# Attention scores from two row groups of the array instead of zero-padded key copies

## The chip, the cores and the metric

The kernel runs on one core of a Trainium2 chip. A core has TensorE (PE, matrix products), VectorE (DVE), ScalarE (ACT), GpSimd (POOL) and SyncE (SP, which here issues nearly all transfers). They run side by side and meet through semaphores. The metric is the device time of one execution in microseconds, the median of several.

## The reference

Three stages, all in fp32. `cur` is linear attention with a decaying state, for 2 batches, 8 heads, 768 positions and head size 48; its result goes as 1536 tokens of 384 features through a gated layer with 8 experts (hidden size 1024, top one, capacity 384) and then through a dense layer of hidden size 2048 with a squared relu.

```python
for t in range(S):
    kt, vt, rt = (k[:, :, t], v[:, :, t], r[:, :, t])
    cur = np.einsum('bhd,bhe->bhde', u[None] * kt, vt)
    y[:, :, t] = np.einsum('bhd,bhde->bhe', rt, state + cur)
    state = w[None, :, :, None] * state + np.einsum('bhd,bhe->bhde', kt, vt)
...
h = np.maximum(np.einsum('ecd,edf->ecf', disp, w1), 0.0)
y = np.einsum('ecf,efd->ecd', h, w2)
...
out = (np.maximum(x @ w_in, 0.0) ** 2) @ w_out
```

## The kernel before

**The attention loop.** The sequence is cut in chunks of C = 128 positions. A loop of three iterations with four steps each (`SLOTS = 4`) goes over 12 chunks, n = 0 to 11, that alternate between the two batches. The 8 heads stand as G = 4 pairs: of a pair g, head o=0 lies in partitions 0 to 47 and head o=1 in partitions 64 to 111 (`D = 48`, `ODD = 64`, `ROWS = 112`); the partitions between hold zeros. Each step works in a slot of its own for its inputs; `am`, `ps_a0`, `ps_a1`, `ps_y` and `ps_kv` exist once, `Kb` and `vb` twice.

One step n does this, engine by engine:

- SP stores the result of chunk n-4, waits for that store to land (`x_stored`), and then issues the loads of chunk n: `feat` (queries and keys by feature), `vT`, `rk` and `vx` (L280 to L283). The first four chunks and two weight pieces are issued ahead of the loop, and SP's queue is in order.
- POOL multiplies the keys in `feat` by their decay in place (L360, `k_decayed`), then the queries into `Rd` (L361, `r_decayed`), then makes `khat` (L367) and `ru` (L369).
- ACT copies the keys of the two heads of each pair to `Kb` (`kb_ready`), where the other head's rows stay zero; then the gate's logits to `vx`, the values to `vb`, and the decayed state to `Sd`.
- PE computes the values' gate products (L427, 3 matmuls), the scores (L433, 8 matmuls of 112 rows, 128x128 each, pair by pair), the state update `ps_kv` (L441, 4 matmuls) and the output `ps_y` (L449 and L451, 12 matmuls: state part, then one masked score block per head, accumulated).
- DVE masks each bank of scores into `am` (L795, with the triangle `before`), makes `ru`, `csum` and `cv` (L799 to L802), adds `ps_y` and `cv` into `x_sb` (L805) and `heads_l` (L806), updates the state (L811) and sums the router's logits (L814).

A bank of scores holds four blocks of 128 columns. Before, bank 0 holds both heads of pairs 0 and 1, bank 1 both heads of pairs 2 and 3. PE signals `scored` after each bank, DVE signals `masked` after each, and the y phase waits for the first before pairs 0 and 1 and for the second before pairs 2 and 3. All matmuls are in fp32; each appears in the trace as two instructions. Engines run their instructions in program order, and the next step's gate products and scores are behind this step's y phase on PE.

**After the loop** DVE, PE and POOL compute the routing (L830 on), POOL gathers the tokens of each expert from `attention_out`, and the expert stage and the dense stage follow, on weights streamed by SP.

Ahead of the loop DVE and POOL each clear one `Kb`, and ACT's loop waits for both (`kb_cleared`).

Of the kernel before, what the change touches and what calls it, by code (L numbers as in the profile page):

```python
# [20 lines left out]
P = 128  # L21
F32 = mybir.dt.float32
# [8 lines left out]
B, H, S, D = 2, 8, 768, 48  # L31
# [3 lines left out]
C = 128  # L35
NC_ = S // C
NT = B * NC_
G = H // 2
ODD = 64
ROWS = ODD + D  # L40
# [18 lines left out]
def build(nc, feat_d, vT_d, rk_d, vx_d, w_d, u_d, wg_d, wts_d, xd, out):  # L59
    with ExitStack() as ctx:  # L60
        def sem(name):
            return ctx.enter_context(nc.semaphore(name))

        def sb(name, shape, dt=F32, scope=ctx):
            return scope.enter_context(nc.sbuf_tensor(name, shape, dt))
# [30 lines left out]
        start = sb("start", [P, E])  # L96
# [13 lines left out]
        with ExitStack() as a:  # L110
            feat = [sb(f"feat{u}", [P, 2, G * C], F32, a) for u in range(SLOTS)]
            rk = [sb(f"rk{u}", [P, 2, DM], F32, a) for u in range(SLOTS)]
            vx = [sb(f"vx{u}", [P, H, DX], F32, a) for u in range(SLOTS)]
            vT = [sb(f"vT{u}", [P, KT, C], F32, a) for u in range(SLOTS)]
            Rd = [sb(f"Rd{u}", [P, G * C], F32, a) for u in range(SLOTS)]
            Kb = [sb(f"Kb{u}", [P, G, 2, C], F32, a) for u in range(2)]
            vb = [sb(f"vb{u}", [P, G, 2, 2 * DX], F32, a) for u in range(2)]
            khat = [sb(f"khat{u}", [P, G, P], F32, a) for u in range(SLOTS)]
            ru = [sb(f"ru{u}", [P, DM], F32, a) for u in range(SLOTS)]
            x_sb = [sb(f"x_sb{u}", [P, DM], F32, a) for u in range(SLOTS)]  # L120
            am = sb("am", [P, 2, G * C], F32, a)
            csum = sb("csum", [P, H], F32, a)
            cv = sb("cv", [P, H, DX], F32, a)
            heads_l = sb("heads_l", [P, H, E], F32, a)
            St = [sb(f"St{b}", [P, G, 2 * DX], F32, a) for b in range(B)]
            Sd = sb("Sd", [P, G, 2 * DX], F32, a)
            T = sb("T", [P, G, 256], F32, a)
            Tk = sb("Tk", [P, G, C], F32, a)
            Tr = sb("Tr", [P, G, C], F32, a)
            iw = sb("iw", [P, G], F32, a)  # L130
            wcol = sb("wcol", [P, G], F32, a)
            tokw = sb("tokw", [P, G, P], F32, a)
            ub = sb("ub", [P, DM], F32, a)
# [15 lines left out]
        ps_a = [ps_a0, ps_a1]  # L149
# [25 lines left out]

        k_decayed = sem("k_decayed")
        r_decayed = sem("r_decayed")
        kb_cleared = sem("kb_cleared")
        kb_ready = sem("kb_ready")
        sd_ready = sem("sd_ready")  # L180
        khat_ready = sem("khat_ready")
        ru_ready = sem("ru_ready")
# [3 lines left out]
        scored = sem("scored")  # L186
        masked = sem("masked")
# [68 lines left out]
        def chunk_view(ap):  # L256
            return ap.rearrange("p (g s) -> p g s", g=G)
# [68 lines left out]
        def _(pool):  # L326
# [10 lines left out]
            def iota(dst, pattern, base, mult):  # L337
# [13 lines left out]
            steps.after(nc.gpsimd.memset(earlier[:, :, :], 1.0))  # L351
            nc.gpsimd.affine_select(out=earlier[:, :, :], in_=earlier[:, :, :], compare_op=ALU.is_gt, fill=0.0, base=0,
                                    pattern=[[1, E], [-1, E]], channel_multiplier=0).then_inc(consts, 1)
            nc.gpsimd.memset(Kb[1][:, :, :, :], 0.0).then_inc(kb_cleared, 1)
            pool.wait_ge(table_ready, 1)
            with pool.Fori(0, NC_ // 2) as i:
                for u in range(SLOTS):
# [52 lines left out]
        def _(pe):  # L410
# [3 lines left out]
            for g in range(G):  # L414
                mm = pe.transpose(ps_kv[:, g * P:g * P + ROWS], Tr[0:ROWS, g, :], ident[0:ROWS, 0:ROWS])
# [4 lines left out]
            with pe.Fori(0, NC_ // 2) as i:  # L420
                for u in range(SLOTS):
                    n, b = 4 * i + u, u % 2

                    pe.wait_ge(in_vT[u], 16 * (i + 1))
                    pe.wait_ge(vx_ready, n + 1)
                    for k in range(KT):
                        mm = pe.matmul(ps_x[:, 0:H * E], vT[u][:, k, :], wg[:, k, :], start=(k == 0), stop=(k == KT - 1))  # L427
                    mm.then_inc(vwg_psum, 1)
                    pe.wait_ge(kb_ready, 2 * n + 2)
                    pe.wait_ge(r_decayed, n + 1)  # L430
                    for g in range(G):
                        for o in range(2):
                            mm = pe.matmul(ps_a[g // 2][:, (2 * (g % 2) + o) * C:(2 * (g % 2) + o + 1) * C],  # L433
                                           Kb[u % 2][0:ROWS, g, o, :], Rd[u][0:ROWS, g * C:(g + 1) * C], start=True, stop=True)
                        if g % 2:
                            mm.then_inc(scored, 1)
                    pe.wait_ge(khat_ready, n + 1)
                    pe.wait_ge(vx_ready, n + 2)
                    pe.wait_ge(state_ready, 2 * n + 2)
                    for g in range(G):  # L440
                        mm = pe.matmul(ps_kv[0:ROWS, g * 2 * DX:(g + 1) * 2 * DX], khat[u][:, g, 0:ROWS],  # L441
                                       vx[u][:, 2 * g:2 * g + 2, :].rearrange("p o d -> p (o d)"), start=True, stop=True)
                    mm.then_inc(kv_done, 1)
                    pe.wait_ge(vb_ready, 2 * n + 2)
                    for g in range(G):
                        if g % 2 == 0:
                            pe.wait_ge(masked, 2 * n + g // 2 + 1)
                        pair = ps_y[:, g * 2 * DX:(g + 1) * 2 * DX]
                        pe.matmul(pair, Rd[u][0:ROWS, g * C:(g + 1) * C], St[b][0:ROWS, g, :], start=True, stop=False)  # L449
                        for o in range(2):  # L450
                            mm = pe.matmul(pair, am[:, g // 2, (2 * (g % 2) + o) * C:(2 * (g % 2) + o + 1) * C],  # L451
                                           vb[u % 2][:, g, o, :], start=False, stop=(o == 1))
                    mm.then_inc(y_done, 1)

# [4 lines left out]
            for j in range(1, NT + 1):  # L459
                mm = pe.matmul(ps_pos[:, 0:nt], ones_b[:, :], oh[:, NT - j:2 * NT + 1 - j, :].rearrange("p t e -> p (t e)"),  # L460
                               start=False, stop=(j == NT))
            mm.then_inc(pos_psum, 1)

            for t in range(NT):
                pe.wait_ge(onehot, t + 1)
                mm = pe.matmul(ps_tab[:, 0:2 * E * CT], onehb[:, t, :], tokb[:, t, :, :].rearrange("p a s -> p (a s)"),
                               start=(t == 0), stop=(t == NT - 1))
# [55 lines left out]
            for q in range(CT):  # L523
                pe.wait_ge(first_gathered[q], 16)
                for k in range(KT):
                    mm = pe.transpose(ps_e[k][:, q * P:(q + 1) * P], xg[0][:, q, k * P:(k + 1) * P], ident[:, :])
# [94 lines left out]
        def _(act):  # L621
            def copy(dst, src):
                return nc.scalar.activation(dst, src, ACT.Copy)  # L623
# [1 line left out]
            act.wait_ge(tokw_psum, 1)  # L625
            copy(tokw[:, :, 0:ROWS], chunk_view(ps_kv[:, :])[:, :, 0:ROWS]).then_inc(tokw_ready, 1)

            act.wait_ge(kb_cleared, 2)
            with act.Fori(0, NC_ // 2) as i:
                for u in range(SLOTS):  # L630
                    n, b = 4 * i + u, u % 2

                    act.wait_ge(k_decayed, n + 1)
                    for o in range(2):
                        rows = slice(ODD * o, ODD * o + D)
                        copy(Kb[u % 2][rows, :, o, :], chunk_view(feat[u][rows, 1, :])).then_inc(kb_ready, 1)
                    act.wait_ge(in_tok[u], 32 * (i + 1))
                    act.wait_ge(vwg_psum, n + 1)
                    copy(vx[u][:, :, D:DX], ps_x[:, 0:H * E].rearrange("p (h e) -> p h e", h=H)).then_inc(vx_ready, 1)
                    act.wait_ge(vx_ready, n + 2)  # L640
                    act.wait_ge(vb_cleared, 2)
                    values = vx[u][:, :, :].rearrange("p (g o) d -> p g o d", o=2)
                    for o in range(2):
                        copy(vb[u % 2][:, :, o, o * DX:(o + 1) * DX], values[:, :, o, :]).then_inc(vb_ready, 1)

                    act.wait_ge(state_ready, 2 * n + 2)
                    for g in range(G):
                        nc.scalar.activation(Sd[0:ROWS, g, :], St[b][0:ROWS, g, :], ACT.Copy,
                                             scale=T[0:ROWS, g, 192:193]).then_inc(sd_ready, 1)
# [94 lines left out]
        def _(dve):  # L744
            v = nc.vector
# [4 lines left out]

            v.memset(T[w, :, 64:65], 1.0)
            v.memset(oh[:, :, :], 0.0).then_inc(vx_ready, 1)
            v.memset(Kb[0][:, :, :, :], 0.0).then_inc(kb_cleared, 1)
            dve.wait_ge(in_w, 16)
            v.tensor_copy(T[w, :, 65], wcol[w, :]).then_inc(dve_step, 1)
            v.reciprocal(T[w, :, 63], wcol[w, :]).then_inc(dve_step, 1)
# [3 lines left out]
            while m <= 128:  # L760
                top = min(64 + 2 * m, 255)
                n = top - 64 - m
# [26 lines left out]
            with dve.Fori(0, NC_ // 2) as i:  # L789
                steps.enter(i, 5 * SLOTS)  # L790
                for u in range(SLOTS):
                    n, b = 4 * i + u, u % 2
# [16 lines left out]
                    for o in range(2):  # L809
                        rows, cols = slice(ODD * o, ODD * o + D), slice(DX * o, DX * o + DX)  # L810
# [228 lines left out]
```

## Time and profile before

| | us |
|---|---|
| median of 3 runs | 480.9 |
| lowest and highest run | 480.21, 481.16 |
| profiled execution, from its first to its last instruction (span) | 477.0 |
| PE busy in the span | 433.4 |
| DVE busy | 294.8 |
| ACT busy | 218.9 |
| POOL busy | 119.7 |

The profiled execution's own time is given as its span alone; the median of the runs is 3.9 us above it. The profile lists instructions with their start and duration, and for an idle engine what it waited for. Each group of matmuls on PE is pipelined, so the rows of consecutive groups overlap by the time that one instruction takes to pass; what counts is the distance of the starts. The granted clock is a share of 2.4 GHz.

### The profile page before, as it was taken

What the parts mean: (1) busy time and instruction counts of PE and PEld (TensorE: products, weight loads), DVE (VectorE), ACT (ScalarE), POOL (GpSimd) and SP (SyncE); (2) the same over time, 40 slices, a digit from 0 to 9 for tenths busy, and PEclk for the clock granted to TensorE, in tenths of its full rate; (3) what the DMA queues carried; (4) which work ended last, traced back from release to release, by engine and by line L of the source; (5) the groups of instructions that cost most, each with busy time, mean ns of one, the idle gap of its engine ahead of it and who ended that gap; (6) DMA issues with size and microseconds to landing.
All of it is one profiled execution on the core that took longest, in us unless ns stands there. A gap on an engine that the chain in (4) does not pass through costs nothing.

```text
span 477.0 us, 8640 instructions
## 1 busy us (share of the span) xinstructions
PE 433.4 (91%) x2933; PEld 408.4 (86%) x2934; DVE 294.8 (62%) x490; ACT 218.9 (46%) x382; POOL 119.7 (25%) x114
## 2 busy tenths in 40 slices
PE   2998989525999999999999999999999999999993
PEld 2998988514999999999899889898998989899892
DVE  8888877689467666676666574554635455553431
ACT  2554544321456647556555463444544345544320
POOL 6955765556940220220000000000300000300003
PEclk9999999955899999999999999999999999999998
DMA  7966576770375475465354423232522313400001
GB/s 212 299 219 207 172 239 209 287 264 26 117 234 191 156 226 196 159 223 198 135 198 154 181 88 111 71 129 67 160 104 81 117 66 132 133 0 1 0 0 67
DMA packets 20989, 69.51 MB, mean 146 GB/s; under 512 B 3352, under 2 KB 9769, under 8 KB 20960
## 3 DMA queue, kind: packets, MB, share of 16 engines
q1 hardware_dynamic: 18656, 64.40, 41.5%
q0 software_dynamic: 2304, 4.73, 2.7%
q8 instruction: 18, 0.29, 0.2%
q14 instruction: 11, 0.09, 0.1%
HBM read 64.39 MB, written 7.08 MB: 150 GB/s over the span
## 4 chain that ended last, share of the span: by engine, by line
PE 76%; DMA 9%; DVE 6%; issue 3%; SPq 3%; POOL 1%; ACT 0%; ACTq 0%; DVEq 0%; POOLq 0%
PE bank L482 36%; PE bank L501 21%; PE bank L491 14%; DMA attention_out<-x_sb 8%; PE bank L473 1%; DVE osb L894 1%; PE bank L433 1%; DMA vx<-in_vx 1%; PE bank L451 1%; DVE r_q L848 1%; SPq L280 1%; SPq L281 1%; SPq L282 1%; SPq L283 1%; DVE r_q L847 0%
## 5 line engine op out<-in xcount | busy, mean ns | idle before, releaser
L900 DVE TENSOR_TENSOR wlo<-raw,whi 128x1536 fp32r<-128x1536 f32 x53 | 93.2, 1758 | 99.9 <-ACT whi L623 99.6
L623 ACT ACTIVATE whi<-raw 128x1536 fp32r<-128x1536 f32 x56 | 83.1, 1488 | 85.3 <-PE bank L501 46.7
L403 POOL DMA_INDIRECT out<-osb,oidx x12 | 12.9, 1076 | 246.2 <-ACT osb L735 243.8
L501 PE MATMUL bank<-whi,hhi 128*128 128x384 f32 x192 | 64.7, 337 | 0.2 <-DVE hlo L919 0.2
L501 PE MATMUL bank<-whi,hlo 128*128 128x384 f32 x192 | 64.7, 337 | 0.0
L501 PE MATMUL bank<-wlo,hhi 128*128 128x384 f32 x192 | 64.6, 336 | 0.0
L482 PE MATMUL bank<-yhi,wlo 128*128 (+1 forms) x144 | 56.9, 395 | 0.0
L482 PE MATMUL bank<-yhi,whi 128*128 (+1 forms) x144 | 56.8, 394 | 0.0
L482 PE MATMUL bank<-ylo,whi 128*128 (+1 forms) x144 | 56.8, 394 | 0.0
L482 PE MATMUL bank<-xshi,whi 128*128 128x256 f32 x192 | 55.3, 288 | 1.1 <-DVE xslo L904 0.9
L491 PE MATMUL bank<-hhi,whi 128*128 128x256 f32 x192 | 55.5, 289 | 0.2 <-DVE ylo L949 0.2
L482 PE MATMUL bank<-xslo,whi 128*128 128x256 f32 x192 | 54.5, 284 | 0.9 <-issue 0.9
L482 PE MATMUL bank<-xshi,wlo 128*128 128x256 f32 x192 | 54.3, 283 | 0.0
L491 PE MATMUL bank<-hlo,whi 128*128 128x256 f32 x192 | 53.6, 279 | 0.0
L491 PE MATMUL bank<-hhi,wlo 128*128 128x256 f32 x192 | 53.6, 279 | 0.0
L676 ACT ACTIVATE rl<-bank 128x512 f32<-128x512 f32 x48 | 28.6, 601 | 53.8 <-PE bank L482 53.8
L915 DVE TENSOR_TENSOR sq<-rl 128x512 f32<-128x512 f32 x48 | 32.9, 688 | 29.9 <-ACT rl L676 29.9
L389 POOL DMA_INDIRECT xg<-attention_out,gidx x24 | 24.8, 1034 | 74.0 <-PE bank L473 60.6
L482 PEld LDWEIGHTS bank<-xshi,whi 128*128 128x128 f32 x192 | 36.8, 192 | 2.6 <-DVE xslo L904 2.1
L482 PEld LDWEIGHTS bank<-xslo,whi 128*128 128x128 f32 x192 | 36.9, 192 | 1.1 <-issue 1.1
L501 PEld LDWEIGHTS bank<-whi,hhi 128*128 128x128 f32 x192 | 36.1, 188 | 1.6 <-issue 0.6
L501 PEld LDWEIGHTS bank<-wlo,hhi 128*128 128x128 f32 x192 | 36.1, 188 | 1.0
(153 smaller groups left out, 861.2 us busy)
## 6 DMA issues: line engine op xcount, KB each, us to landing
raw<-in_wts SPq DMA_DIRECT2D x56, 768.0 KB, 4.3
feat<-in_feat SPq DMA_DIRECT2D x12, 448.0 KB, 3.9
rk<-in_rk SPq DMA_DIRECT2D x12, 384.0 KB, 4.5
vx<-in_vx SPq DMA_DIRECT2D x12, 224.0 KB, 5.2
vT<-in_vT SPq DMA_DIRECT2D x12, 192.0 KB, 3.8
attention_out<-x_sb SPq DMA_DIRECT2D x12, 192.0 KB, 4.6
out<-xg SPq DMA_DIRECT2D x12, 192.0 KB, 2.3
xg<-attention_out,gidx POOLq DMA_INDIRECT x24, 3.6
```

The lines of the kernel that those rows point to most:

```text
L280: sp.dma_start(feat[u][0:ROWS, :, :], feat_d[b, bass.ds(c, 1)].rearrange("a p k n -> (a p) k n")).then_inc(in_feat[u], 16)
L281: sp.dma_start(vT[u][:, :, :], vT_d[b, bass.ds(c, 1)].rearrange("a p k s -> (a p) k s")).then_inc(in_vT[u], 16)
L282: sp.dma_start(rk[u][:, :, :], rk_d[b, bass.ds(c, 1)].rearrange("a s k n -> (a s) k n")).then_inc(in_tok[u], 16)
L389: nc.gpsimd.indirect_dma_start(out=xg[e % 2][:, q, :], out_offset=None, in_=xd[:, :], in_offset=bass.IndirectOffsetOnAxis(ap=gidx[:, e * C ...
L403: nc.gpsimd.indirect_dma_start(out=out[:, :], out_offset=bass.IndirectOffsetOnAxis(ap=oidx[:, t:t + 1], axis=0), in_=osb[:, t, :], in_offs ...
L482: mm = pe.matmul(banks[ft][:, 0:width], w[:, r, cols], x(k), start=(k == 0 and step == 0), stop=(k == KT - 1 and step == 2))
L491: mm = pe.matmul(ps_e[dt][:, 0:width], w[:, r, cols], x[:, par, ft, 0:width], start=(q == 0 and ft == 0 and step == 0), stop=(q == EQ - 1 ...
L501: mm = pe.matmul(ps_o[tt][:, 0:DM], x[:, par, ft, tt * P:(tt + 1) * P], w[:, r, cols], start=(v == 0 and ft == 0 and step == 0), stop=(v = ...
L623: return nc.scalar.activation(dst, src, ACT.Copy)
L676: nc.scalar.activation(rl[:, ft, :], banks[ft][:, :], ACT.Relu).then_inc(h_relu, 1)
L900: v.tensor_tensor(wlo[:, r, :], raw[:, r, :], whi[:, r, :].bitcast(F32), ALU.subtract).then_inc(w_lo, 1)
L915: v.tensor_tensor(sq[:, ft, :], rl[:, ft, :], rl[:, ft, :], ALU.mult).then_inc(h_sq, 1)
```

## The change

The scores of the head o of a pair are computed from its own 48 rows alone: the stationary operand is the keys in `feat` and the moving one `Rd`, both cut to rows 0 to 47 or 64 to 111. Bank o now holds the heads o of all four pairs, and the mask and the y phase read the blocks by that order. `Kb`, ACT's two copies a step and the two clears go. PE waits for POOL's `k_decayed` itself, both `scored` signals come at the last pair, and the y phase waits for both masks before its first matmul.

```diff
-            Kb = [sb(f"Kb{u}", [P, G, 2, C], F32, a) for u in range(2)]
...
-            nc.gpsimd.memset(Kb[1][:, :, :, :], 0.0).then_inc(kb_cleared, 1)
...
-                    pe.wait_ge(kb_ready, 2 * n + 2)
+                    pe.wait_ge(k_decayed, n + 1)
                     pe.wait_ge(r_decayed, n + 1)
                     for g in range(G):
                         for o in range(2):
-                            mm = pe.matmul(ps_a[g // 2][:, (2 * (g % 2) + o) * C:(2 * (g % 2) + o + 1) * C],
-                                           Kb[u % 2][0:ROWS, g, o, :], Rd[u][0:ROWS, g * C:(g + 1) * C], start=True, stop=True)
-                        if g % 2:
-                            mm.then_inc(scored, 1)
+                            rows = slice(ODD * o, ODD * o + D)
+                            mm = pe.matmul(ps_a[o][:, g * C:(g + 1) * C], feat[u][rows, 1, g * C:(g + 1) * C],
+                                           Rd[u][rows, g * C:(g + 1) * C], start=True, stop=True)
+                            if g == G - 1:
+                                mm.then_inc(scored, 1)
...
                     pe.wait_ge(vb_ready, 2 * n + 2)
+                    pe.wait_ge(masked, 2 * n + 2)
                     for g in range(G):
-                        if g % 2 == 0:
-                            pe.wait_ge(masked, 2 * n + g // 2 + 1)
                         pair = ps_y[:, g * 2 * DX:(g + 1) * 2 * DX]
                         pe.matmul(pair, Rd[u][0:ROWS, g * C:(g + 1) * C], St[b][0:ROWS, g, :], start=True, stop=False)
                         for o in range(2):
-                            mm = pe.matmul(pair, am[:, g // 2, (2 * (g % 2) + o) * C:(2 * (g % 2) + o + 1) * C],
+                            mm = pe.matmul(pair, am[:, o, g * C:(g + 1) * C],
                                            vb[u % 2][:, g, o, :], start=False, stop=(o == 1))
...
-            act.wait_ge(kb_cleared, 2)
...
-                    act.wait_ge(k_decayed, n + 1)
-                    for o in range(2):
-                        rows = slice(ODD * o, ODD * o + D)
-                        copy(Kb[u % 2][rows, :, o, :], chunk_view(feat[u][rows, 1, :])).then_inc(kb_ready, 1)
...
-            v.memset(Kb[0][:, :, :, :], 0.0).then_inc(kb_cleared, 1)
```

## Rows read from the trace of the kernel before

**Rows 1.** The page: chain of work that ended last, by engine and by line

```profile
PE 76%; DMA 9%; DVE 6%; issue 3%; SPq 3%; POOL 1%; ACT 0%; ACTq 0%; DVEq 0%; POOLq 0%
PE bank L482 36%; PE bank L501 21%; PE bank L491 14%; DMA attention_out<-x_sb 8%; PE bank L473 1%; DVE osb L894 1%; PE bank L433 1%; DMA vx<-in_vx 1%; PE bank L451 1%; DVE r_q L848 1%; SPq L280 1%; SPq L281 1%; SPq L282 1%; SPq L283 1%; DVE
```

**Rows 2.** SP's queue in order of time: start us, us, operation

```profile
19.19 0.36 SPq L288 DMA_DIRECT2D attention_out<-x_sb  x1
28.28 0.35 SPq L280 DMA_DIRECT2D feat<-in_feat  x1
...
30.46 0.35 SPq L288 DMA_DIRECT2D attention_out<-x_sb  x1
...
79.11 0.34 SPq L280 DMA_DIRECT2D feat<-in_feat  x1
```

**Rows 3.** SP's waits up to 100 us: total us, times, longest

```profile
SPq L280 <- DMA attention_out<-x_sb: 39.4, 8, 8.5
```

**Rows 4.** DVE in order of time: start, steps 1 and 2, 6, 11

```profile
2.48 0.17 DVE L755 COPY T<-wcol 112x4 f32<-112x4 f32 x1 [0.32 <-DMA wcol<-in_w]
...
24.36 0.56 DVE L805 TENSOR_TENSOR x_sb<-bank,cv 128x384 f32<-128x384 f32 x1
...
26.42 1.29 DVE L795 TENSOR_TENSOR am<-bank,before 128x512 f32<-128x512 f32 x2
...
30.30 0.56 DVE L805 TENSOR_TENSOR x_sb<-bank,cv 128x384 f32<-128x384 f32 x1 [0.79 <-PE bank L451]
...
56.44 0.56 DVE L805 TENSOR_TENSOR x_sb<-bank,cv 128x384 f32<-128x384 f32 x1
...
86.76 0.69 DVE L795 TENSOR_TENSOR am<-bank,before 128x512 f32<-128x512 f32 x1 [0.72 <-PE bank L433]
...
91.19 0.56 DVE L805 TENSOR_TENSOR x_sb<-bank,cv 128x384 f32<-128x384 f32 x1 [1.04 <-PE bank L451]
```

**Rows 5.** POOL in order of time, steps 0 and 11

```profile
5.71 1.50 POOL L360 TENSOR_TENSOR feat<-feat,Tk 112x512 f32<-112x512 f32 x1 [1.00 <-DMA feat<-in_feat]
...
82.93 1.27 POOL L360 TENSOR_TENSOR feat<-feat,Tk 112x512 f32<-112x512 f32 x1 [2.44 <-DMA feat<-in_feat]
84.16 1.26 POOL L361 TENSOR_TENSOR Rd<-feat,T 112x512 f32<-112x512 f32 x1
```

**Rows 6.** ACT in order of time, step 11

```profile
84.23 1.28 ACT L623 ACTIVATE Kb<-feat 48x512 f32<-48x512 f32 x2 [3.71 <-POOL feat L360]
```

**Rows 7.** PE in order of time, step 11

```profile
85.56 2.05 PE L433 MATMUL bank<-Rd,Kb 112*128 112x128 f32 x16 [0.94 <-ACT Kb L623]
87.45 0.95 PE L441 MATMUL bank<-vx,khat 128*112 128x112 f32 x8
88.24 0.39 PE L449 MATMUL bank<-St,Rd 112*128 112x112 f32 x2
```

**Rows 8.** PE in order of time, step 2, which waits for no load

```profile
24.09 0.79 PE L427 MATMUL bank<-wg,vT 128*128 128x64 f32 x6
24.72 2.00 PE L433 MATMUL bank<-Rd,Kb 112*128 112x128 f32 x16
26.56 0.95 PE L441 MATMUL bank<-vx,khat 128*112 128x112 f32 x8
```

**Rows 9.** PE in order of time, the first step

```profile
11.02 3.73 PE L433 MATMUL bank<-Rd,Kb 112*128 112x128 f32 x16
14.54 1.10 PE L441 MATMUL bank<-vx,khat 128*112 128x112 f32 x8
15.47 0.39 PE L449 MATMUL bank<-St,Rd 112*128 112x112 f32 x2
```

**Rows 10.** Windows (us): engines' busy time, granted clock, DMA share, GB/s

```profile
26.00:28.00 2.00, 2.00 (x21) 2.00 (x20) 1.85 (x4) 1.95 (x6) 1.28 (x2) 1.00 0.37 146
28.00:29.00 1.00, 1.00 (x11) 1.00 (x10) 0.84 (x3) 0.42 (x1) 0.00 (x0) 1.00 0.00 0
```

**Rows 11.** A window at the start of the expert stage

```profile
120.00:124.00 4.00, 3.86 (x20) 3.86 (x21) 0.93 (x5) 0.39 (x2) 3.69 (x3) 0.58 0.60 239
```

More of the change, by code:

```diff
@@ L177, in build @@
         r_decayed = sem("r_decayed")
-        kb_cleared = sem("kb_cleared")
-        kb_ready = sem("kb_ready")
         sd_ready = sem("sd_ready")
```

## The prediction

> **What bounds the kernel now.** I read the page first, its chain of work, to see where the changed loop stands in the whole [rows 1]. TensorE holds 76% of the chain, but nearly all of that is the expert and MLP stage, where the change touches nothing. The attention loop ends at about 91 us of 477.0, and its own entry in the chain is a transfer: the stores of attention_out take 8% of the span. The second view is SyncE's queue in order of time, and who it waits for [rows 2, 3]. From the first finished chunk on, SP does the same round eight times: issue the store of chunk n, wait for its landing, issue the four loads of chunk n+4, go on to store n+1. It waited 39.4 us for landings in 8 waits, 4.9 each. The rounds run from 19.19 to 79.11, 7.5 us apart on average ((79.11 - 19.19)/8). The results are ahead of SP: that of chunk 1 was there at 24.9 (its x_sb began at 24.36 [rows 4]) and SP came to it at 30.46; that of chunk 6 was there at 57.0, and at the mean round SP comes to it some ten microseconds later. So in the middle of the loop the compute engines follow the loads, and a faster or slower step there buys or costs nothing so long as the results stay ahead of SP.
>
> That leaves two places where a step still counts. One is the last chunk, n=11. Its features were issued at 79.11, and POOL decayed keys and queries from 82.93 to 85.42 [rows 5]. ACT copied the keys to Kb until 85.51 [rows 6], the first score matmul began at 85.56, kv at 87.45, the first y matmul at 88.24 [rows 7], and DVE took the result at 91.19 [rows 4]. What follows (routing, gather, experts) hangs on that moment. The other is the period of a step that does not wait for a load, since a backlog could reach the last chunk. The steady step shows it: x_sb began at 24.36 and 30.30, a period of 5.94 us [rows 4]. TensorE is full in it (gate 0.63, scores 1.84, kv 0.78, y the remaining 2.69; starts from [rows 8]), and DVE's own circle is as long: x_sb to the first mask 2.06 us, then about 0.69 for half of the masking, then y.
>
> **The change part by part.** *Kb's copies go.* ACT's two copies, 1.28 us a step, ended 0.09 us after POOL had Rd ready (85.51 against 85.42 [rows 5, 6]). The step can begin only that much sooner, 0.08 us (85.56 becomes about 85.48), because POOL's second multiplication is late next. ACT's freed time buys nothing more: it holds 0% of the chain [rows 1].
>
> *The two clears of Kb go* (128x1024 on DVE and on POOL ahead of the loop). Behind its clear DVE still sat 0.32 us idle for the transfer of `wcol` [rows 4], and POOL 1.00 us for the first features [rows 5], so I cost both at nothing; without that cover each is worth what a clear takes, 0.9 us. SP's queue and all transfers stay as they are.
>
> *The scores.* The number of matmuls stays: 8 a step, in the trace 16 instructions. Before, they are 0.118 us apart (87.45 - 85.56 over 16) and one lasts d = 2.05 - 15 x 0.118 = 0.28 us [rows 7]. What half the rows cost, no row shows: every matmul of the trace uses 112 or 128 rows. The two ends: (a) the two heads' instructions do not overlap, pitch 0.118 as before; (b) two heads run at once, a pair of matmuls per 0.236 us where it was 0.47. The nearest rows speak for both. Gate matmuls stream 64 columns, half of the scores' 128, and still come every 0.105 us [rows 8] (0.63/6); so something other than the streaming, presumably the weight load ahead of each, keeps 0.10 us per instruction, and if loads of the two row groups stand in one line, (a) holds. Against that, the two groups share neither rows nor a bank. I take (b), narrowly, and keep (a) for the range.
>
> The Trainium skill, TensorEngine Tiling (Array Packing), Key Properties, says that different tiles can load and multiply in parallel, which would be (b); no row here shows it. TensorE: Matmul & The Clock Gate, LDWEIGHTS, of the same Trainium skill, says that a load costs by its columns and not by its rows; the 0.105 us at 64 streamed columns agrees with a floor of that sort, and by that rule alone the sum would be that of (a).
>
> *The masks.* Before, the first bank held four head blocks and was complete after half of the scores, so DVE masked it while TensorE wrote the second. Now the heads alternate and the bank of the first heads is complete only at the 14th of 16 instructions; and y waits for both masks where it waited for one. Before, the first mask began 0.09 us after the eighth instruction's end (85.56 + 7 x 0.118 + 0.28 = 86.67, mask at 86.76 [rows 4]). Two masks back to back take 1.29 us [rows 4] (26.42). From the end of a copy to the waiting matmul it is 0.05 us (85.51 to 85.56). Behind the waiting y stand y's 24 instructions and the next chunk's gate and scores; DVE's x_sb waits for them.
>
> The last step then:
> - (b): 85.48 + 3 x 0.236 + 0.118 + 0.28 + 0.09 = 86.68; masks to 87.97; y at 88.02, against 88.24. Gain 0.2 us. kv no longer stands between, it runs beside the masks: POOL's khat is there at about 86.6, kv's 0.79 end at 87.4.
> - (a): 85.48 + 13 x 0.118 + 0.28 + 0.09 = 87.38; masks to 88.67; y at 88.72. Loss 0.5 us.
>
> The break-even pitch lies between, nearer to (b): 0.7 us of scores saved are met by 0.5 us of masking that was hidden.
>
> *The first step* works on a slower TensorE: 16 instructions in 3.52 us, 0.22 apart, d = 3.73 - 15 x 0.22 = 0.43 [rows 9]. Under (b) the first x_sb comes up to 0.9 us sooner, under (a) 15.74 - 15.47 = 0.27 later, and SP's first store with it. It moves no load: the DMA engines are busy until about 28 with what SP had queued before, the first chunks and two weight pieces (share 0.37 from 26 to 28, zero from 28 to 29 [rows 10]), and the store that went out at 19.19 was seen as landed just before 28.28 [rows 2]. It stands behind those bytes either way.
>
> *The backlog.* The period without loads becomes, by DVE's circle, 2.06 + 1.29 + 0.05 + 2.95 (y to x_sb, 91.19 - 88.24) = 6.35 us under (b). Under (a) the scores come into it: they start 0.36 after x_sb (24.72 - 24.36), so 0.36 + 1.53 + 0.28 + 0.09 + 1.29 + 0.05 + 2.95 = 6.55. Both are under SP's 7.5. From the first x_sb at 18.4 (15.47 + 2.95), 11 periods end at 18.7 + 72.1 = 90.8 even under (a), before the 91.7 that the last load allows. The cover is 0.9 us there, and 2 us or more under (b).
>
> The sum on the profiled execution: span 477.0 becomes 476.8 under (b), 477.5 under (a). The median of the runs, 480.9, is 3.9 us above the span, and I carry that over.
>
> **The rivals.**
> - A, (b) as above: 480.9 - 0.2 = 480.7 us.
> - B, the row groups do not overlap, so that the change does not do what it says: 480.9 + 0.5 = 481.4 us. For it: the 0.105 us of the gate matmuls [rows 8]. Against: the operands are disjoint.
> - C, slower: the second mask in the chain makes a backlog that reaches the last chunk. DVE's steps were longer than 5.94 even before: from 24.36 to 56.44 they took 32.08 us for 5, 6.42 each [rows 4], 2.4 us in all that DVE lost beside POOL. If all of it comes on top of period 6.55, the last x_sb is at 90.8 + 2.4 = 93.2 instead of 91.2, 2.0 us late; it decides once more than 0.9 us of it isn't absorbed. Against: these delays fall on work that waits for y anyway, and y now comes 0.6 us later. I set its time at 482.4, three quarters of the full price.
> - D, faster: the earlier first store does start the loads earlier. All eight rounds and the last load move by up to 0.9 us, and with A's 0.2 that is 479.8 us. Against: the busy DMA engines until 28 us [rows 10].
> - E, the clock: before, it stands at 2.4 GHz in the loop [rows 10], and before the last scores TensorE idles 0.94 us [rows 7], and the expert stage's first matmuls run at a mean of 0.58 of it [rows 11]. With scores at half their time TensorE idles more, and the rise in the expert stage may fall elsewhere. A microsecond either way, 479.9 to 482.
>
> **How the numbers follow.** About 0.2% (1.0 us) is what the measurement tells from no change, the three runs spread over 0.95 us. Chances: A 0.42, B 0.32, C 0.13, D 0.05, E 0.08. The forecast is A, 480.7 us. The range must hold A, B and most of C: 479.9 to 482.4. Same (479.9 to 481.9) holds A, most of B and half of E: 0.73. Slower: C, with a share of E and of B, whose 481.4 lies 0.5 below the bound: 0.19. Faster: D and the rest: 0.08.
>
> **What would show it.** A: in the last step the 16 score instructions span about 1.2 us instead of 2.05; the two masks follow each other without a gap; y starts 2.5 to 2.6 us after POOL's Rd (it was 2.8). B: they span 2.05 us and y starts 3.3 us after. C: TensorE does not wait for POOL in the last chunks, and x_sb is over 6 us behind Rd. D: the first landing that SP sees is before 28.1. SP's rounds otherwise stay 7.5 us apart and its wait for landings near 39 us. I am wrong if switching between row groups and the full array costs more than the pitches here, if SP's rounds drift apart or together by a microsecond, or if TensorE's rate in the loop falls to the first step's 0.22 us.

## The result, and the profile after

The changed kernel is slower: 484.6 us (median of 6 runs) against 480.57 for the kernel before (6 runs), ratio 1.0084 with the 95% interval 1.0052 to 1.0116. The forecast was 480.7 us, no change, with a range up to 482.4. The profiled execution has a span of 481.4 us where it was 477.0. Both are traces of short executions. The changed kernel's took 483.08 us, the least of its six. An execution takes 1.7 to 2.9 us more than its span in all runs here that have both, so the 477.0 of before belong to one of about 479 us, some 2 us under that kernel's median.

The first view is SP's queue of the changed kernel in order of time, to be held against [rows 2].

```profile
17.98 0.37 SPq L285 DMA_DIRECT2D attention_out<-x_sb  x1
29.77 0.36 SPq L277 DMA_DIRECT2D feat<-in_feat  x1
...
31.95 0.35 SPq L285 DMA_DIRECT2D attention_out<-x_sb  x1
...
81.07 0.34 SPq L277 DMA_DIRECT2D feat<-in_feat  x1
```

The first store went out 1.2 us earlier, and its landing was seen 1.5 us later. From there on SP's rounds are about as long as before (7.1 to 7.6 us, 7.3 on average; before 6.4 to 7.5, 7.3 on average), and the last features are issued at 81.07 instead of 79.11. Step 11 follows, by POOL, PE and DVE in order of time ([rows 4, 5, 7] before).

```profile
86.02 1.27 POOL L357 TENSOR_TENSOR Rd<-feat,T 112x512 f32<-112x512 f32 x1
```

```profile
87.44 1.16 PE L430 MATMUL bank<-Rd,feat 48*128 48x128 f32 x16 [1.01 <-POOL Rd L357]
88.53 1.04 PE L438 MATMUL bank<-vx,khat 128*112 128x112 f32 x8
90.03 0.45 PE L445 MATMUL bank<-St,Rd 112*128 112x112 f32 x2 [0.47 <-DVE am L785]
```

```profile
23.73 0.56 DVE L795 TENSOR_TENSOR x_sb<-bank,cv 128x384 f32<-128x384 f32 x1 [0.69 <-PE bank L447]
...
30.23 0.56 DVE L795 TENSOR_TENSOR x_sb<-bank,cv 128x384 f32<-128x384 f32 x1 [1.12 <-PE bank L447]
...
88.60 1.29 DVE L785 TENSOR_TENSOR am<-bank,before 128x512 f32<-128x512 f32 x2 [0.76 <-PE bank L430]
...
93.04 0.56 DVE L795 TENSOR_TENSOR x_sb<-bank,cv 128x384 f32<-128x384 f32 x1 [1.35 <-PE bank L447]
```

The reader is to see three things. The 16 score instructions take 1.16 us instead of 2.05: the two row groups do run at once. Behind them PE now waits 0.47 us for the masks. And from the end of Rd to x_sb it is 93.04 - 87.29 = 5.75 us, before 91.19 - 85.42 = 5.77: the shorter scores and the longer wait cancel. The period without loads is 6.50 (30.23 - 23.73) where it was 5.94.

So in this pair of traces x_sb of the last chunk is 1.85 us late because the loads are. The other part of the loss lies where the change touches nothing, behind the loop. DVE writes the index table `gidx`. POOL gathers the first expert's tokens with it (an indirect transfer), then computes the low part of weight piece 2 (`split_lo(2)`, called the split below), while DVE builds a second table (`tokv`) and twelve one-hot matrices for the token places (`osb` in the rows, which shares its memory). PE multiplies the first six of these, turns the gathered tokens, and starts the experts. DVE, POOL and PE of the kernel before:

```profile
107.35 0.18 DVE L866 TENSOR_SCALAR gidx<-off 128x24 uint32<-128x24 f32 x1
...
111.98 0.31 DVE L889 TENSOR_TENSOR tokv<-tokv,tokid 128x144 f32<-128x144 f32 x1
112.33 6.37 DVE L894 TENSOR_SCALAR osb<-iota_p,r_pc 128x128 f32<-128x128 bf16 x12
```

```profile
110.86 1.23 POOL L389 DMA_INDIRECT xg<-attention_out,gidx  x1 [8.28 <-issue]
...
114.76 3.45 POOL L376 TENSOR_TENSOR wlo<-raw,whi 128x1536 fp32r<-128x1536 f32 x1
```

```profile
120.14 0.39 PE L482 MATMUL bank<-xshi,whi 128*128 128x256 f32 x1 [0.90 <-DVE xslo L904]
```

The same of the changed kernel:

```profile
109.21 0.18 DVE L856 TENSOR_SCALAR gidx<-off 128x24 uint32<-128x24 f32 x1
...
113.93 4.12 DVE L879 TENSOR_TENSOR tokv<-tokv,tokid 128x144 f32<-128x144 f32 x1
118.09 2.44 DVE L884 TENSOR_SCALAR osb<-iota_p,r_pc 128x128 f32<-128x128 bf16 x12
```

```profile
110.37 1.23 POOL L385 DMA_INDIRECT xg<-attention_out,gidx  x1 [5.95 <-DVE gidx L856]
...
114.44 3.44 POOL L372 TENSOR_TENSOR wlo<-raw,whi 128x1536 fp32r<-128x1536 f32 x1
```

```profile
124.91 0.39 PE L478 MATMUL bank<-xshi,whi 128*128 128x256 f32 x1
```

POOL's first gather came 3.33 us after the end of gidx before (110.86 - 107.53) and comes 0.98 us after it now (110.37 - 109.39). POOL is 2.3 us faster there, and that is what hurts. Its split now comes upon the last product of `tokv`, which takes 4.12 us instead of 0.31 and ends 0.17 us behind the split's end (118.05 against 117.88). By its row the product began 0.5 us ahead of the split's (113.93 against 114.44), under POOL's third gather; that it is the split which holds it is shown by experiment 4. Not one of the one-hots is there before 118. Before, the split hit DVE in the middle of the one-hots, and PE had its first six. The first expert matmul comes 15.5 us behind gidx instead of 12.6. Summed: 1.85 (loads) + 0.01 (routing up to gidx) + 2.91 (gather to experts) - 0.37 (from the first expert matmul to the end) = 4.4 us, the difference of the spans. The first experts ran at half clock from 122 to 124 us before (granted 0.50) and at full clock from 124 us on now.

That DVE and POOL hold each other up is what the Trainium skill, SBUF — State Buffer, Terms, says of the port pair that they share: it is held for a whole instruction, and the other blocks. The 4.12 us for a product that takes 0.31 without the split agree. The same shows inside the loop already before the change: DVE's `cv` product (128x448) takes 0.62 us in most steps, and 2.82 us at 34.85, beside POOL's multiplications.

### The profile page after: what moved, and what is told of

Read it like the earlier page. It is cut to its first block, busy times and chain, and to the rows that moved or that the text cites. A ratio compares the mean times of both kernels' runs of the same rounds, so it can differ in the third digit from the quotient of the medians.

```text
span 481.4 us, 8599 instructions
## 1 busy us (share of the span) xinstructions
PE 429.0 (89%) x2933; PEld 400.4 (83%) x2934; DVE 289.5 (60%) x489; ACT 204.5 (42%) x358; POOL 118.0 (25%) x113
## 4 chain that ended last, share of the span: by engine, by line
PE 77%; DMA 10%; DVE 5%; issue 3%; SPq 2%; POOL 1%; ACT 0%; DVEq 0%; POOLq 0%
PE bank L478 35%; PE bank L497 21%; PE bank L487 14%; DMA attention_out<-x_sb 8%; PE bank L469 2%; DMA vx<-in_vx 1%; PE bank L515 1%; DVE tokv L879 1%; PE bank L447 1%; DVE r_q L838 1%; PE bank L430 1%; SPq L277 1%; SPq L278 1%; SPq L279 1%; SPq L280 1%
## 5 line engine op out<-in xcount | busy, mean ns | idle before, releaser
L487 PEld LDWEIGHTS bank<-hhi,whi 128*128 128x128 f32 x192 | 36.1, 188 | 0.1
```

Source lines behind the costliest of these rows:

```text
L487: mm = pe.matmul(ps_e[dt][:, 0:width], w[:, r, cols], x[:, par, ft, 0:width], start=(q == 0 and ft == 0 and step == 0), stop=(q == EQ - 1 ...
```

## Experiments

Theories after the result: **F**, the length of POOL's instruction stream (the sequence of its instructions) decides whether its first gather stalls, since a piece of program has to be fetched there; **P**, the collision of the split with DVE's table is what a prompt gather costs; **L**, the late loads are chance of one execution; **H**, the loop itself costs something through drops of TensorE's clock.

**1. Both kernels again**, unchanged.

> The kernel before, unchanged, for a second trace. All theories: the same time, ratio 1.00 within 0.3%. What it tells apart is in the trace. Theory L (the lateness of the changed kernel's loads is chance of one execution): the first landing that SP sees moves between 28.3 and 30 us from trace to trace of one and the same kernel. Theory F (a fetch of instructions stalls POOL at its first gather, at a place in its instruction stream): POOL's first gather comes again 3.3 us after the index table, as in the first trace.

> The changed kernel, unchanged, for a second trace; ratio about 1.008. Theory P (the attention loop ends 1.9 us late, and behind it a collision of POOL's split of weight piece 2 with DVE's table costs 2.5 us more): last x_sb about 1.9 us later than before, the first expert matmul over 4 us later, POOL's first gather within 1 us of the index table. Rival: the loss is one execution's chance, and the second trace shows the loop's end within 0.5 us of before.

Ratios 1.0017 (0.999 to 1.0045) and 1.008 (1.0061 to 1.0099). SP's queue and POOL of the kernel before, second trace:

```profile
30.34 0.35 SPq L280 DMA_DIRECT2D feat<-in_feat  x1
```

```profile
112.60 1.23 POOL L389 DMA_INDIRECT xg<-attention_out,gidx  x1 [8.16 <-issue]
```

L holds as to the loads: the unchanged kernel saw its first landing at 30.3 in one trace and at 28.3 in the other, and its last x_sb came at 93.07, as late as the changed kernel's 93.04 and 93.19. So the 1.85 us of the first pair of traces need not be the change's doing. The gather's lag does not vary so: 3.2 us behind gidx here, and 1.0 us again in the changed kernel. This second pair has its loops end together, and its spans, 481.9 and 479.1, still differ: 0.12 (the last x_sb) + 3.24 (the first expert matmul 15.73 us behind gidx against 12.49) - 0.56 (from there to the end) = 2.8 us. The stretch behind the first expert matmul lies between 355.2 and 357.7 us in all fourteen traces, so a sum over one pair is good to about a microsecond.

**2. Kb kept, the clear moved.** The changed kernel with the two buffers still allocated and cleared, and the kernel before with POOL's clear done by DVE:

```diff
-            nc.gpsimd.memset(Kb[1][:, :, :, :], 0.0).then_inc(kb_cleared, 1)
...
-            v.memset(Kb[0][:, :, :, :], 0.0).then_inc(kb_cleared, 1)
+            for u in range(2):
+                v.memset(Kb[u][:, :, :, :], 0.0).then_inc(kb_cleared, 1)
```

> The changed kernel with the two Kb buffers allocated and cleared as before, but neither written nor read in the loop. If addresses or the length of POOL's instruction stream make the loss (theory F), the time returns to that of before plus at most 0.3 us, ratio 0.999 to 1.001, and POOL's first gather stalls 3.3 us behind the table. If the scores, masks and ACT's missing copies make it, the ratio stays at 1.007 to 1.009.

> The kernel before with POOL's clear of the second Kb moved to DVE, so that POOL's stream is as long as in the changed kernel; nothing in the loop differs. Theory F: the stall of POOL's gather vanishes (first gather within 1 us of the table), POOL's split of piece 2 meets DVE's table, and the time rises by 2 to 3 us (ratio 1.004 to 1.007). Rival (the loop's own edits make the loss): ratio 1.00.

Kb kept: 1.004 (1.0008 to 1.0072), between F's forecast and the rival's, and right by neither. Two of its twelve executions took 486.7 and 487.0 us, the other ten 479.3 to 483.9; the mean of the ten is 1.002 of the kernel before. In its trace the gather is at 112.15, 3.2 us behind gidx, and the first expert matmul 12.5 us, as in the kernel before. Clear moved, with a loop that is that of before: 1.0069 (1.0044 to 1.0094), or 1.006 without the one execution of 488.3 us. POOL and DVE of the latter:

```profile
109.34 1.23 POOL L388 DMA_INDIRECT xg<-attention_out,gidx  x1 [5.94 <-DVE gidx L866]
...
113.43 3.43 POOL L375 TENSOR_TENSOR wlo<-raw,whi 128x1536 fp32r<-128x1536 f32 x1
```

```profile
117.07 2.44 DVE L894 TENSOR_SCALAR osb<-iota_p,r_pc 128x128 f32<-128x128 bf16 x12
```

The gather is prompt (0.97 us), the one-hots start only behind the split. One clear less on POOL, far ahead of the loop, makes nearly the whole loss without the rest of the change.

**3. A filler on POOL.** One clear of 128x8 elements that nobody reads, where Kb's clear was, in the changed kernel and, as one instruction more, in the kernel before:

```diff
+            nc.gpsimd.memset(filler[:, :], 0.0).then_inc(filled, 1)
             pool.wait_ge(table_ready, 1)
```

> The changed kernel with one tiny clear (128x8 of a scratch tensor that nobody reads) put on POOL where the clear of Kb had been. Theory F (the place of a fetch in POOL's instruction stream decides): POOL's first gather comes 3.2 to 3.3 us after the index table again, DVE has finished the one-hots' first half before POOL's split of piece 2, and the time is that of before within 0.3% (ratio 1.000 to 1.003). Rival (the length of the clear, or Kb's addresses, mattered): the lag stays at 1.0 us and the ratio at 1.007 to 1.009.

> The kernel before with one tiny clear more on POOL. Theory F in its simple form (one instruction less frees the gather, one more keeps the fetch in its way): the gather stays 3.2 us behind the table, ratio 1.00 within 0.3%. If the stall has an edge on this side too, the gather comes 1.0 us behind the table and the ratio rises to about 1.007.

The changed kernel with the filler: 1.0007 (0.998 to 1.0034), the loss is gone to within 0.3%, although scores, masks and the missing copies are those of the changed kernel. POOL and DVE:

```profile
112.43 1.23 POOL L388 DMA_INDIRECT xg<-attention_out,gidx  x1 [8.16 <-issue]
...
116.34 3.46 POOL L375 TENSOR_TENSOR wlo<-raw,whi 128x1536 fp32r<-128x1536 f32 x1
```

```profile
113.98 6.31 DVE L887 TENSOR_SCALAR osb<-iota_p,r_pc 128x128 f32<-128x128 bf16 x12
```

The kernel before with one more: 1.0059 (1.0026 to 1.0091), and the gather is prompt:

```profile
109.07 1.23 POOL L392 DMA_INDIRECT xg<-attention_out,gidx  x1 [5.95 <-DVE gidx L869]
```

Theory F in its simple form (less frees it, more keeps it) falls: of the three lengths tried the stall exists at one, and one instruction either way ends it. What fills the stall shows in the DMA view of the time between gidx and gather, before (107.6 to 110.9 us):

```profile
DMA packets 1, 0.01 MB, mean 2 GB/s; under 512 B 0, under 2 KB 0, under 8 KB 0
...
q14 instruction: 1, 0.01, 0.9%
```

and of the changed kernel (109.5 to 110.4):

```profile
DMA packets 0, 0.00 MB, mean 0 GB/s; under 512 B 0, under 2 KB 0, under 8 KB 0
```

One packet of the queue that carries instructions lies in the gap in all eight traces with the stall, 1.1 to 1.4 us behind the end of gidx, and the gather starts 2.0 to 2.2 us behind it; none lies in the gap of the six traces with a prompt gather. There it has moved: with one instruction less it comes 0.8 to 1.1 us behind the gather's start (at 111.15 us in the changed kernel), and with one more it came 4.6 us ahead of the end of gidx, in the kernel before with the filler (103 to 104 us):

```profile
q14 instruction: 1, 0.01, 1.9%
```

That this packet is POOL's, and that POOL waits for it, is argued from these places and from the edits, not shown by a semaphore. The Trainium skill, Runtime: NRT & Kernel Launch, Instruction fetch mechanics, says that instructions are fetched ahead in sequence and that a taken branch out of the present window stalls the engine; POOL runs a loop of three iterations ahead of this gather, and by that rule the place of a fetch depends on where each instruction lies. The traces agree as far as one instruction moves it; that a branch is to blame no run shows.

**4. The split behind the one-hots**, in both kernels and in the kernel with the clear moved:

```diff
                 if e == 0:
+                    pool.wait_ge(onehot, 2 * NT)
                     split_lo(2)
```

> The changed kernel, but POOL waits for DVE's twelve token one-hots (24 signals of onehot) before it splits weight piece 2. Theory P (the collision of that split with DVE's table costs it): DVE's last table product takes 0.3 us instead of 4.1, the one-hots run unstalled, the first expert matmul comes about 12.5 us or less behind the index table instead of 15.6, and the ratio falls from 1.008 to between 0.998 and 1.002. Rival (the late place is lost elsewhere, as the split now ends later and the first expert matmul waits for it): ratio 1.005 or more.

> The kernel before with the same wait. Here the one-hots come before the split's end anyway. Theory P: DVE's one-hots take 2.4 instead of 6.3 us, but the split starts no earlier than at present, so the first expert matmul moves by less than 1 us either way; ratio 0.996 to 1.003. With the collision gone from both, this and the changed kernel with the same wait differ by under 0.2%; if the loop's own edits cost time, they differ by more.

> The kernel before with POOL's clear moved to DVE (1.0069 alone) and POOL waiting for the token one-hots ahead of its split of piece 2; the loop is that of before. Theory F with P (the early gather costs only through the collision): the first gather stays 1.0 us behind the index table, DVE's one-hots run unstalled, the first expert matmul comes 11.6 us or less behind the table instead of 16.1, ratio 0.997 to 1.001. Rival (moving the clear costs in some other way): the ratio stays above 1.004.

Ratios 1.0025 (0.999 to 1.006), 1.0001 (0.9973 to 1.0028) and 1.0025 (1.0 to 1.0051). DVE, POOL and PE of the changed kernel with the wait:

```profile
114.55 0.31 DVE L880 TENSOR_TENSOR tokv<-tokv,tokid 128x144 f32<-128x144 f32 x1
114.90 2.44 DVE L885 TENSOR_SCALAR osb<-iota_p,r_pc 128x128 f32<-128x128 bf16 x12
```

```profile
117.42 3.44 POOL L372 TENSOR_TENSOR wlo<-raw,whi 128x1536 fp32r<-128x1536 f32 x1 [2.59 <-DVE osb L885]
```

```profile
121.72 0.39 PE L479 MATMUL bank<-xshi,whi 128*128 128x256 f32 x1 [0.36 <-DVE xslo L895]
```

The collision is gone, the first expert matmul comes 11.7 us behind gidx (110.01) instead of 15.5, and about two thirds of the loss with it, at the prompt gather. P holds as to the collision; the ratio of 1.0025 lies just above its forecast of at most 1.002, and its interval (0.999 to 1.006) reaches from no loss to the rival's 1.005. In the kernel before the same wait brought the first expert matmul to 11.6 us behind gidx from 12.6, and no time (1.0001), so this lag does not turn into time one for one. The kernel with the clear moved stayed above its forecast of at most 1.001; its trace ends the loop late for a reason of its own (below). No version beats the kernel before.

**5. Both masks before y**, alone in the kernel before:

```diff
+                    pe.wait_ge(masked, 2 * n + 2)
                     for g in range(G):
-                        if g % 2 == 0:
-                            pe.wait_ge(masked, 2 * n + g // 2 + 1)
```

> The kernel before with y waiting for both masks ahead of its first matmul, scores and Kb as they were. Prediction's step (the second mask is on the path): in a step that waits for a load, x_sb comes 0.2 to 0.4 us later behind Rd than the 5.76 us of before (the second mask ends at 88.34, y began at 88.24), and the unloaded period grows from 5.94 to over 6.3 us; the time rises by at most 0.1%. Rival (a backlog reaches the last chunk): over 6.5 us behind Rd and 0.3% or more.

```profile
24.35 0.56 DVE L804 TENSOR_TENSOR x_sb<-bank,cv 128x384 f32<-128x384 f32 x1 [0.82 <-PE bank L450]
...
30.85 0.56 DVE L804 TENSOR_TENSOR x_sb<-bank,cv 128x384 f32<-128x384 f32 x1 [1.28 <-PE bank L450]
...
93.69 0.56 DVE L804 TENSOR_TENSOR x_sb<-bank,cv 128x384 f32<-128x384 f32 x1 [1.36 <-PE bank L450]
```

The step is as expected: 6.06 us behind Rd (87.63) instead of 5.77, period 6.50. The time is not: 1.0047 (1.0013 to 1.008) where I had at most 0.1%. The trace shows no backlog in the last step, and behind the loop it has the lags of the kernel before (gather 3.4 us, first expert matmul 12.5). The lower end of the interval comes near 0.1%; what would make more than that stays open, the more so as the changed kernel has this same edit and costs 1.0007 with the filler.

**6. TensorE kept busy.** The changed kernel with the filler and the state matmuls done a second time into a bank nobody reads (work that is not part of the result):

```diff
                     mm.then_inc(kv_done, 1)
+                    for g in range(G):
+                        pe.matmul(ps_tab2[0:ROWS, g * 2 * DX:(g + 1) * 2 * DX], khat[u][:, g, 0:ROWS],
+                                  vx[u][:, 2 * g:2 * g + 2, :].rearrange("p o d -> p (o d)"), start=True, stop=True)
```

> The changed kernel with POOL's filler (ratio 1.0007 alone) and TensorE doing the four state matmuls of each step twice, the second time into a bank that nobody reads, in the time in which it waits for the masks. Theory H (the drops of the clock inside the loop come from TensorE's idle time there): no stretch at half clock inside the loop, last x_sb within 6.0 us of the last Rd, ratio 0.998 to 1.002, although work was added. Rival (the drops are chance, or the added 0.8 us is on the path): the period without loads grows beyond 6.7 us or the clock drops again, ratio above 1.003.

1.0044 (1.0012 to 1.0075). The period stayed at 6.5, the added work was hidden, and the clock fell all the same. Windows of this kernel, then of the changed kernel with the late split, then of the kernel with the clear moved and the late split (granted clock third from the end):

```profile
69.00:73.00 4.00, 4.00 (x25) 4.00 (x25) 3.17 (x5) 0.84 (x4) 3.93 (x4) 0.57 0.40 126
```

```profile
44.00:48.00 4.00, 4.00 (x21) 4.00 (x20) 0.64 (x3) 0.00 (x0) 1.80 (x2) 0.50 0.90 290
```

```profile
71.00:81.00 10.00, 9.61 (x47) 9.43 (x46) 5.81 (x11) 4.18 (x12) 8.01 (x8) 0.52 0.60 190
```

At a granted clock of 0.50 (1.2 GHz) y took 5.2 us in the second of these traces (41.97 to 47.19), and 2.7 at full clock in its next step (51.08 to 53.82); at a period of 6.5 the loop may not catch up. The last x_sb came 10.2, 8.8 and 10.3 us behind Rd in these three traces instead of 5.76, and 6.5 in that of the changed kernel with the filler alone. H's forecast for this run missed, and the third of these kernels has the loop of before. But H itself isn't refuted, because the doubled matmuls did not fill the idle time that stood ahead of the fall. DVE and PE of this run:

```profile
64.10 2.82 DVE L798 TENSOR_TENSOR cv<-vx,csum 128x448 f32<-128x448 f32 x1
```

```profile
68.64 1.15 PE L441 MATMUL bank<-vx,khat 128*112 128x112 f32 x8 [1.61 <-DVE St L807]
```

DVE's product ran long beside POOL, the state came late, and TensorE stood idle for 1.61 us ahead of the state matmuls, first and doubled ones alike; the clock fell within the next microsecond. In every trace with a fall inside the loop TensorE had idled shortly before, 1.3 us or more in one wait, or twice about half a microsecond (changed kernel, second trace). Idle time is not enough for it: waits of 1.35 us (both masks) and 1.74 us (clear moved) passed without a fall. A drop inside the loop shows in 2 of the 6 traces with the loop of before and in 6 of the 7 with the changed loop, the profiled one among them (granted clock 0.50 from 66 to 68 us). That leans towards the change and is too few traces to settle.

**7. Both cures.** The changed kernel with the filler and the late split.

> The changed kernel with both cures: POOL's filler (stall of the gather kept) and POOL waiting for the token one-hots ahead of its split of piece 2. If nothing but the two places behind the loop separates the changed kernel from the one before, it is as fast as the kernel before with the same wait (1.0001): ratio 0.997 to 1.002, first gather 3.2 us and first expert matmul 11.6 us behind the index table. If the loop's own edits cost 0.2% or more, the ratio is above 1.002.

1.0019 (0.9993 to 1.0046), against 1.0001 for the kernel before with the same late split. The gather comes 3.2 us and the first expert matmul 12.1 us behind gidx, where I had 11.6. Whether the loop's edits cost 0.2% or nothing cannot be told from this.

## Why the prediction was wrong

The loop was read rightly in the main. The row groups overlap (1.16 us; I had about 1.2). The masks follow without a gap and are on the path. The store that went out 1.2 us earlier brought no load forward. The last step's gain of 0.2 us came out as 0.02 (y began 2.74 us behind Rd, not 2.60), because the lags from POOL's Rd to PE and from DVE's mask to PE were about 0.15 us each where I had 0.05, and y to x_sb took 3.01 instead of 2.95. The same two sizes make the period 6.5 instead of 6.35. My 7.5 us for SP's rounds took in the first, longer wait; from load to load they are 7.3 apart. These are small sizes.

The step that failed is the pricing of the clears: "I cost both at nothing; without that cover each is worth what a clear takes, 0.9 us". I counted the duration of POOL's clear and not that it is one instruction of POOL's stream. Taking it out brought POOL's first gather from 3.2 to 1.0 us behind gidx, and its split onto DVE's table. Moving that clear alone to DVE gave 1.0069, and putting back a clear of 128x8 brought the changed kernel to 1.0007. With it fell "What follows (routing, gather, experts) hangs on that moment": the stretch behind the loop did not shift with its start, it grew by 2.9 us up to the first expert matmul (3.2 in the second pair). None of the rivals had this place. C, the slower one, named a backlog. Its mechanism occurs (four traces above, one of them with the loop of before, each behind a fall of the clock), but in the profiled pair the last chunk was bound by its load in both kernels.

I also took one trace's load times for the kernel's. The first landing moved by 2 us between two traces of the same program, ten times the gain of 0.2 us that the forecast took from the last step of one of them. And I carried over 3.9 us from span to median, of which some 2 us are only that the profiled execution was a fast one; the difference that I forecast does not hang on that.

## What to carry to other kernels

An edit that adds or drops one instruction ahead of an engine's loop can move a stall behind that loop; when a small change costs what no step of it explains, compare the lags between the same pairs of instructions in both traces, far behind the edit, and try one filler instruction before believing in the edit's own cost. An engine that arrives earlier is no gain where it shares something with the engine on the path: order such a piece of work by a wait on what it must not disturb. Before a difference of some tenths of a microsecond is priced, a second trace of the same kernel tells how far its transfers move by themselves. And before a run is said to refute a cause, its own trace should show that the edit removed that cause.

## What the hardware showed unexpectedly

- fp32 matmuls of 48 rows in two row groups, each with its own load of 128 columns, took 1.16 us for 16 instructions where 112 rows took 2.05. The gate matmuls' 0.105 us at 64 streamed columns was no floor for this.
- A POOL gather stalled 2.2 to 2.4 us at one of the three lengths of POOL's program that were tried, with one packet of the instruction queue in the gap.
- A DVE product of 128x144 elements took 4.12 us instead of 0.31 with POOL's split beside it.
- The granted clock fell to 0.50 inside the loop behind idle waits of TensorE of no more than 1.75 us each, in eight of fourteen traces.
